# One move of the attention output earlier on ScalarE, and one SBUF copy earlier in SyncE's queue

## The reference

```
q_bits = (q @ proj > 0);  k_bits = (k @ proj > 0)
mask   = (q_bucket[:, None] == k_bucket[None, :])
scores = where(mask, q @ k.T / sqrt(64), -1e9)
attn   = exp(scores - max);  attn = attn / (sum(attn) + 1e-9);  o = attn @ v
```

## Time and profile before

| what | us |
|---|---|
| median of 3 runs (lowest, highest) | 1006.72 (1006.39, 1007.02) |
| the profiled execution's own time | 1006.95 |
| its span, first to last instruction | 1005.2 |
| PE busy in the span | 987.0 (98%) |
| POOL busy in the span | 443.9 (44%) |
| attention, about | 0 to 239 |

### The profile page before, as it was taken

How to read it: one execution, slowest core, us unless ns; L and a number is a source line. 1 busy time by engine, 2 the same in 40 slices (tenths; PEclk the granted TensorE clock), 3 DMA queues, 4 the chain that set the end, 5 groups by cost and what they waited for, 6 DMA issues and landing times.

```text
span 1005.2 us, 16461 instructions
## 1 busy us (share of the span) xinstructions
PE 987.0 (98%) x5408; PEld 911.3 (91%) x5408; DVE 672.9 (67%) x1119; ACT 462.6 (46%) x849; POOL 443.9 (44%) x436
## 2 busy tenths in 40 slices
PE   7999999999999999999999999999999999999998
PEld 5989999998899999999888989989889898898987
DVE  6888888887855555555896555665555655556555
ACT  4887888888444344344543323223232232322321
POOL 3677779998565373554633404123041230412100
PEclk9999999999999999999999999999999999999999
DMA  5566566662101002010020100101002010020002
GB/s 137 154 168 169 164 178 168 177 160 80 37 22 43 22 21 63 21 42 21 22 63 22 43 22 21 63 21 42 21 21 63 21 42 21 21 63 21 21 20 105
DMA packets 50724, 65.40 MB, mean 65 GB/s; under 512 B 5408, under 2 KB 32128, under 8 KB 50688
## 3 DMA queue, kind: packets, MB, share of 16 engines
q1 hardware_dynamic: 50528, 64.58, 22.9%
q10 hardware_dynamic: 160, 0.39, 0.1%
HBM read 44.07 MB, written 3.19 MB: 47 GB/s over the span
## 4 chain that ended last, share of the span: by engine, by line
PE 89%; DVE 5%; issue 2%; ACT 2%; DMA 1%; POOL 1%; SPq 1%; DVEq 0%; ACTq 0%
PE ps L1498 32%; PE ps L1521 25%; PE ps L1529 11%; PE ps L1415 6%; PE ps L1445 6%; PE ps L1426 6%; PE ps L1389 2%; DVE xq_lo L1078 1%; DVE xq_raw L1066 1%; DVE hb L1193 0%; DMA q_lo<-k_st 0%; DMA proj_raw<-in_proj 0%; DVE acc L1207 0%; ACT wd_hi L783 0%; DVE acc L1220 0%
## 5 line engine op out<-in xcount | busy, mean ns | idle before, releaser
L1498 PE MATMUL ps<-xq_hi,wu_lo 128*128 128x384 f32 x672 | 227.0, 338 | 2.3 <-DVE xq_lo L1078 1.1
L1498 PE MATMUL ps<-xq_hi,wu_hi 128*128 128x384 f32 x672 | 226.2, 337 | 0.0
L1498 PE MATMUL ps<-xq_lo,wu_hi 128*128 128x384 f32 x672 | 226.1, 336 | 0.0
L1224 DVE SCALAR_TENSOR_TENSOR acc<-ps,p_norm,acc 128x512 f32<-128x512 f32 x180 | 135.0, 750 | 100.9 <-PE ps L1521 95.3
L589 POOL TENSOR_TENSOR wu_lo<-wu_raw,wu_hi 128x768 fp32r<-128x768 f32 (+1 forms) x48 | 103.9, 2186 | 219.0 <-ACT wu_hi L779 219.0
L1521 PE MATMUL ps<-wd_lo,g_hi 128*128 128x512 f32 x384 | 150.9, 393 | 0.0
L1521 PE MATMUL ps<-wd_hi,g_hi 128*128 128x512 f32 x384 | 150.9, 393 | 0.0
L1521 PE MATMUL ps<-wd_hi,g_lo 128*128 128x512 f32 x384 | 150.6, 392 | 0.0
L1498 PEld LDWEIGHTS ps<-xq_hi,wu_lo 128*128 128x128 f32 x672 | 126.1, 188 | 8.4 <-ACT hb L845 1.7
L1498 PEld LDWEIGHTS ps<-xq_lo,wu_hi 128*128 128x128 f32 x672 | 126.2, 188 | 3.9
L924 ACT ACTIVATE g_hi<-hb 128x384 fp32r<-128x384 f32 x96 | 50.5, 526 | 165.5 <-DVE hb L1182 100.7
(11 more groups left out here) (123 smaller groups left out, 1757.1 us busy)
## 6 DMA issues: line engine op xcount, KB each, us to landing
wu_raw<-in_w SPq DMA_DIRECT2D x64, 128.0 KB, 3.0
wd_raw<-in_w SPq DMA_DIRECT2D x16, 512.0 KB, 3.5
q_raw<-in_qT SPq DMA_DIRECT2D x32, 192.0 KB, 3.3
k_raw<-in_kT SPq DMA_DIRECT2D x30, 192.0 KB, 3.3
wu_raw<-in_w_in SPq DMA_DIRECT2D x32, 128.0 KB, 2.3
wd_raw<-in_w_out SPq DMA_DIRECT2D x8, 512.0 KB, 3.7
v_raw<-in_vP SPq DMA_DIRECT2D x16, 192.0 KB, 2.8
inv_rows<-inv_dram SPq DMA_DIRECT2D x16, 192.0 KB, 3.4
```

Source lines behind the costliest of these rows:

```text
L1224: dve.scalar_tensor_tensor(out=part_of, in0=source, scalar=scale, in1=part_of, op0=ALU.mult, op1=ALU.add).then_inc(down_taken, 1)
L1498: mm = pe.matmul(to, w[:, wslot, k, :], x[:, xslot, k, :], start=start and k + m == 0, stop=k == 1 and m == 2, skip_group_check=not start)
```

## The change

Two edits. On SP, `spread_inverse` is split: `store_inverse` is its first part. In every head the order store, wait, read back, shift, key copy becomes store, key copy, wait, read back, shift. In the last pair there is no key copy and the order is as it was. On ACT, in the last pair's step t = 6 (head 15, qt = 0), `move_o(14, 0, 0, 7)` goes from behind `take_exp` to ahead of it.

```diff
+                def store_inverse(h, b):
+                    sp.wait_ge(inv_turn_taken, h + 1)
+                    sp.dma_start(inverse_row(h).rearrange("(t p) -> t p", p=P),
+                                 inv_turned[SLOT * b:SLOT * b + QT, :]).then_inc(inv_stored, 16)
+
                 def spread_inverse(h, b, it):
-                    row = inv_dram[h] if isinstance(h, int) else inv_dram[bass.ds(h, 1)].rearrange("a n -> (a n)")
-                    sp.wait_ge(inv_turn_taken, h + 1)
-                    sp.dma_start(row.rearrange("(t p) -> t p", p=P),
-                                 inv_turned[SLOT * b:SLOT * b + QT, :]).then_inc(inv_stored, 16)
+                    row = inverse_row(h)
                     sp.wait_ge(inv_stored, 16 * h + 16)
...
                         if not at_zero(h):
+                            store_inverse(h - 1, 1 - b)
+                        if exists(h + 2):
+                            spread_beside(h + 2, b)
+                        if not at_zero(h):
                             spread_inverse(h - 1, 1 - b, it)
                             shift_part(h - 1, 1 - b, it if b == 1 else it - 1)
-                        if exists(h + 2):
-                            spread_beside(h + 2, b)
...
+                        if qt == 0 and last and b == 1:
+                            move_o(h - 1, 1 - b, 0, it)
                         if qt == 3 and last and b == 1:
                             move_o(h - 1, 1 - b, 1, it)
                         if not (last and t == TILES - 1):
                             take_exp(i + 1, (t + 1) % TILES)
-                        if qt == 0 and not first:
+                        if qt == 0 and not first and not (last and b == 1):
                             move_o(h - 1, 1 - b, 0, it if b == 1 else it - 1)
```

More of the change, by code:

```diff
@@ L366, in load_v, with inverse_row @@
                     sp.dma_start(v_raw[:], vP[h]).then_inc(v_loaded, 16)
+                def inverse_row(h):
+                    return inv_dram[h] if isinstance(h, int) else inv_dram[bass.ds(h, 1)].rearrange("a n -> (a n)")
+                def store_inverse(h, b):
+                    sp.wait_ge(inv_turn_taken, h + 1)
+                    sp.dma_start(inverse_row(h).rearrange("(t p) -> t p", p=P),
+                                 inv_turned[SLOT * b:SLOT * b + QT, :]).then_inc(inv_stored, 16)
                 def spread_inverse(h, b, it):
-                    row = inv_dram[h] if isinstance(h, int) else inv_dram[bass.ds(h, 1)].rearrange("a n -> (a n)")
-                    sp.wait_ge(inv_turn_taken, h + 1)
-                    sp.dma_start(row.rearrange("(t p) -> t p", p=P),
-                                 inv_turned[SLOT * b:SLOT * b + QT, :]).then_inc(inv_stored, 16)
+                    row = inverse_row(h)
                     sp.wait_ge(inv_stored, 16 * h + 16)
@@ L417, in _ @@
                 pair(PAIRS - 1)
+                store_inverse(HEADS - 1, 1)
                 spread_inverse(HEADS - 1, 1, PAIRS - 1)
```

## The result

The changed kernel took 1012.75 us (median of 6 runs, 1012.33 to 1014.67) against 1006.54 us (6 runs, 1006.23 to 1007.02): ratio 1.0062, 95% interval 1.0051 to 1.0072. It is 6.2 us slower. Forecast were 1008.4 us and a range of 1005.7 to 1010.2, so the time lies outside the range. The direction and the mechanism were right, and the size was not. The profiled execution took 1012.37 us with a span of 1010.6 (before 1006.95 and 1005.2), so 5.4 us of the loss stand in the two traces.

A forecast was written before the change was run, and what follows sets the result against it. PE bounds the kernel, with POOL almost without slack from head 9 on. POOL's lag +2.91, key copy -0.51 and ACT -0.66 sum to +1.74 us: 1008.4 us, range for 8 in 10 1005.7 to 1010.2.

The forecast's parts named there:

- (A): Forecast case: PE pays POOL's lag from head 10 on, net +0.6 to +2.9 us; chance 0.60.
- (C): Rival: landings near 4.5 us, or late `add_eps` holding DVE's inverse; over +2.9, up to 1011 us; chance 0.15.
- (B): Rival: the lag costs less than the gains, by quick shifts or POOL slack; at best 1005.5 us; chance 0.20.
- (D): Rival: an earlier key copy closes PE's gaps ahead of each `bits`; gain 3.4 us, to 1003.3; chance 0.05.
- the landing of the shift, 3.6 us: SP's pv_other transfer, last of four within 2 us, was to land in 3.6 us (3.5 in head 12).
- K: End of POOL's key rounding in a head; pv_other issued at K + 2.0, `x_add` at K + 5.66 us.
- upper bound, 4.48 us: Slow landing of the shift, as last of a packed burst: PE loses 5.6 us, sum +4.4, 1011.1 us.
- 2.45 us: Skill page's landing estimate for a 192 KB GpSimd-issued DMA; the sum would be about -0.9 us, 1005.9.
- up to 2 us later, ... covered: Head 13's first feed-forward weights, up to 2 us later, needed by POOL in head 14 and PE at 239 us: covered.
- the key copy's gain, 0.51 us: PE's wait in head 4 for the key copy goes: gain 0.51 us, bounds 0.5 and 0.7.
- mostly landed 1 us ahead: Argument on PE's gaps ahead of `bits`: the key copy mostly landed 1 us ahead, so it seldom decides.
- ACT's 0.66: Head 15: output move ahead of the exponential, PE released by DVE at 227.59; gain 0.66 us, bounds 0.3 and 0.82.

The follow-up runs named there:

- Experiment 3: Kernel before, with the new SP order in even heads (2 to 12) alone and no ACT edit: 1012.12 us, ratio 1.0049.
- experiment 5: The changed kernel, with POOL's `x_add` moved behind `v_round` and `v_rest` in odd heads: 1007.20 us, ratio 1.0008 to the kernel before.
- 8: Kernel before, both edits undone, with POOL rounding v three more times in heads 9, 11 and 13, no DMA touched: 1012.98 us, ratio 1.0061.
- experiment 4: Kernel before, with the new SP order in odd heads 1 to 11 alone and the ACT edit: 1006.47 us, ratio 0.9999.
- experiment 9: The changed kernel, with only the wait for `k_hi_ready` at the early place and the key copy issued last: 1020.05 us, ratio 1.0138 to before.
- Experiment 6: The changed kernel, with the first feed-forward weights issued ahead of the store in head 13: 1011.19 us, ratio 1.0050 to the kernel before.
- full: The changed kernel with both edits, SP and ACT, against the kernel before: 1012.75 us, ratio 1.0062.
- 10: The changed kernel, with `x_add` behind `v_round` and `v_rest` and the weights ahead of the store in head 13: 1007.01 us, ratio 1.0002 to before.
- Experiment 7: The changed kernel, with the two shifts issued ahead of the read-back of the inverses: 1008.96 us, ratio 1.0023 to the kernel before.

## Why the prediction was right and wrong

**Right: the mechanism and its place.** SP held the shifts behind POOL's rounding, POOL waited at `x_add`, POOL had no slack from head 9 on, and PE waited for `k_rest` ahead of `bits`, most in head 12 (1.83 us; forecast were "about 1.8 us", but for a lag of 2.6 us by then where 3.6 came, so this number agrees in part by luck). POOL's waits at L526 were 1.7 to 2.2 us each, where 1.2 to 1.5 were forecast. Experiment 3 puts it in the even heads, 5 takes it away at POOL, 8 makes it with POOL alone. It was case (A) in kind and (C) in size, whose two conditions both came true, the first in part: landings of 3.9 to 4.3 us where (C) had 4.5, and a late `add_eps` that holds DVE's inverse (3.2 us in 3 waits, each beside a wait of PE for POOL). (B) fell with the first `x_add`. (D) fell with experiment 4 and with `bits` itself: the idle ahead of its weight loads, which (D) said would close, grew from 4.8 us to 7.9.

**Wrong: the landing of the shift, 3.6 us.** This is the term that failed most. From K to `x_add` I had 5.66 us (2.0 to the issue, 3.6, 0.05), in head 12 5.4. The issue was right: head 8's rounding ends at 138.38 and the shift goes out at 140.28, 1.90 later. The landing was 3.9, 4.3 and 4.2 us in heads 8, 10 and 12. So K to `x_add` took 5.92 us in head 8, in head 10, from 168.73 to 175.12, 6.39 us, and in head 12 6.17. Since each turn starts from the last one's lag, the lags are 1.61, 3.71 and 5.48 us where I had 1.43, 2.84 and 3.82, and PE had lost 4.69 us at head 14 where I had 2.91: 1.8 us of the miss. "The burst stays short, so I stay near the median landing" was the sentence that chose it. The median of the earlier trace rows is one of `x_f` and `pv_other` together, sent 1.3 and 1.8 us or so behind the read-back, and the early wait closes that distance to 0.7 and 1.2 us (experiment 9). My own upper bound, 4.48 us from the earlier trace rows, would have given 1011.1. For what the burst does, the Trainium skill (DMA: Bandwidth & Descriptors, "Queues, rings and completion order") says that each DMA engine takes its descriptors in the order of the ring; the landings 2.6, 3.2, 3.5 and 3.9 us agree. The estimate by the same page that the prediction gave, 2.45 us, agrees with the first of them, 2.5 to 2.6 us, and with none behind it.

**Wrong: "up to 2 us later, ... covered", of the weights in head 13.** POOL nearly is: it waits 2.31 us for them, where before it didn't wait. PE isn't: the weights are in the queue when head 15's sign bits are copied, and PE waits 1.06 us. I had listed who needs the weights and not which transfer is behind them. Experiment 6 is 1.6 us under full, 10 is 0.2 under 5, and in both pairs the intervals overlap. In the traces PE's lag grows by 1.30 us at this place in full and by 1.4 in 5, and not in 6 and 10. So it is worth 1 us or so in full; that it is worth less once POOL is in time, as the medians of 5 and 10 say, isn't shown.

**Wrong: the key copy's gain, 0.51 us.** In the pair of traces it is there (73.93 against 74.48 in head 4) and is gone by head 9 (143.92 against 144.00). With the ACT edit alone head 4 starts at 73.93 as well. With the old order in head 3 the wait was 0.51 and 0.24 us in two traces and absent in three, and I priced the largest as a cost of every execution. It isn't a lasting gain, and it should have had a bound of nothing. That the copy "mostly landed 1 us ahead" fits experiment 9: there the copy of head 8 lands 2.1 us later than before, counted from the rounding, and PE waits 0.98 us for it.

**Right: ACT's 0.66.** The idle time went from 0.82 to 0.25 us, 0.57, released by DVE as forecast.

**The sum again**, for the span: 4.69 by head 14, which holds the key copy's nothing, and 1.06 for the weights, less 0.57 for ACT, is 5.18 of 5.4 us. The rest, some 0.2 us, lies in short gaps between head 14's `bits` and the wait for the sign bits. Against the forecast of +1.74, the span's +5.4 is 3.7 us more: 1.8 of the lag, 1.3 of the weights with these gaps, 0.5 of the key copy and 0.1 of ACT.

**What I had overlooked.** Everything that SP issues behind K now bunches up, not only the shift. The copies of the sign bits (L352) land in 4.9, 4.5 and 4.4 us in heads 10, 11 and 12, before in 3.0, and at the scores that need them, starting within 0.2 us of the landing, PE's lag grows by 0.70, 0.43 and 0.24 us. So the 0.47 us in head 10, which the profile puts down to DVE, ended with that copy too. PE's named waits of heads 9 to 14, 0.69, 0.47, 1.83 and 0.75, make 3.7 of its 4.7 us, and these scores hold most of the last microsecond. I take it that they don't add to the end: in heads 12 and 14 PE waits for POOL anyway, and in experiment 5, with landings of 4.2, 4.1 and 4.4 us and POOL in time, PE waits for no such copy. `load_q`, which the prediction called covered, is late as well: POOL waits for it 7.2 us in 4 times, before 1.7 us once, all in heads where it then waits for PE.

**Left open.** No kernel has the early wait with both the key copy and the shift in time, so how the 6.2 us divide between the wait and the transfers ahead isn't measured as a time. Experiment 7, which keeps the wait and brings the shift forward, gives 3.8 of them back. And why a read-back just ahead makes the shift slow no run tells.

## What to carry to other kernels

An issue moved ahead in an in-order queue brings its own wait along. Price it for everything that comes behind it, follow each of these to the engine that needs it, and look there whether that engine, in order too, has slack; here one wait went through SP, a DMA, POOL and PE, and once a lag feeds the next one's start, an error in one duration counts as often as it goes round. A transfer's duration belongs to what is issued just ahead of it: take it from a row with the same transfers at the same distance, not from a median. A short wait in one trace may be half as long or absent in the next, and is not a gain to be had before other traces show it too. And look at the granted clock behind a long wait of TensorE before you put a loss down to anything else.

## What the hardware showed that was not expected

- Of four 192 KB transfers that SP issued within 1.9 us, the landings rose from 2.5 or 2.6 us for the first to 3.9 to 4.3 for the fourth (heads 8, 10 and 12), with the largest step to the second, the read-back: 0.6 to 1.3 us, then 0.2 to 0.4 a transfer.
- The shift landed in 3.9 to 4.4 us with the read-back issued 1.2 us ahead of it, whether it was fourth (full) or third (experiment 9), and in 3.4 or 3.5 us as third with the read-back behind it (experiment 7).
- Behind 1 MB of weights whose issue had ended less than 2 us earlier, and one copy of 192 KB, two copies of 192 KB took 4.7 and 5.6 us to land; with 3.6 us between (before), 2.9 and 3.2.
- After waits of PE of 2.06, 2.03 and 1.93 us (experiments 8, 7 and 3) the granted TensorE clock was 0.50 for some 3 us, and PE's lag grew by 1.6, 1.6 and 1.5 us there without a named wait.
